# Attention and two expert layers on one core: an earlier column of shares, the first six products on ScalarE, sums of x spread over attention steps

## Chip, core and metric

The kernel runs on one core of one Trainium2 chip. The metric is the device time of one execution in microseconds; the time before is the median of three runs. Engines: TensorE (PE, with its weight loads, PEld), VectorE (DVE), ScalarE (ACT), GpSimd (POOL) and SyncE (SP), which issues most of the transfers.

## What is computed

Causal windowed attention with ALiBi-like distances (2 batches, 8 heads, 768 rows, 64 wide) gives x of 1536 x 512. A first expert layer mixes all 8 experts with shares from 8 Sinkhorn steps; a second gives each token to one expert, by rank and with a capacity of 192. This change is about the end of the attention and the start of the first expert layer:

```python
def _moe_ref(x, w_gate, w1, w2):
    logits = x @ w_gate
    logits = logits - logits.max()
    P = np.exp(logits)
    for _ in range(8):
        P /= P.sum(1, keepdims=True) + 1e-09
        P /= P.sum(0, keepdims=True) + 1e-09
        P *= N / E
    out = np.zeros((N, D), dtype=np.float32)
    for e in range(E):
        h = np.maximum(x @ w1[e], 0.0)
        ye = h @ w2[e]
        out += P[:, e:e + 1] * ye
    return out
```

## The kernel before

There is one program for each engine, written out by hand; an engine runs its instructions in the order in which they are written, and semaphores order them between engines.

**Number format.** Products of the first layer use a high and a low part of each operand (`xhi`, `xlo`, `w1hi`, `w1lo`, `hhi`, `hlo`, `w2hi`, `w2lo`): ScalarE casts the high part, VectorE subtracts it for the low part, and `three` on TensorE issues three matmuls (L1561 to L1563) per product.

**Attention.** `attend_window` on each engine is a loop over 48 steps (`STEPS`; 8 heads, 6 row tiles) and seven more that drain it. In step s TensorE makes the scores of s, transposes the probabilities of s-2 and multiplies those of s-3 by v. VectorE adds the bias and takes the row maximum (L1119, `sc`), ScalarE does exp (L711) and copies the transposed probabilities (`pt`, L718). In every third step VectorE also divides finished rows (`x_rows`, L1049 to L1055), and at fixed steps TensorE transposes x and ScalarE copies it (`x_copy`, L655). In the last steps the three engines already prepare the first expert: `w1_sums`, `x_sums` (L1028 to L1034, four sums of quarters of x, `SUMS`; early ones for half k = 0, the other half after the attention), `x_hi` (L664, ScalarE) and `x_lo` (L1011, VectorE), seven parts (`PARTS`) each. They are the operands of a Strassen-like product: seven products of quarters in place of eight.

**First expert layer.** The 1536 tokens go in two halves (`NS`), each expert's 1024 hidden columns in two units: unit u is one half of one expert. For each unit TensorE computes seven parts of h (`h_part`), then six y blocks of 128 tokens x 512 columns (`y_products`, `TS` = 6), of 12 matmuls each. ScalarE's `period` copies three parts out of PSUM (`part_copy`, L758), casts the seven w1 parts of the next unit (`w1_hi`, L752), takes the relu of h (`h_hi`, L767), and casts w2 (`w2_hi`, L738) once all six y of the unit ahead are in PSUM. TensorE's part 2 waits for the first of these copies (`s_rc`). VectorE's `h_period` and `y_period` do the sums and low parts and multiply each y by its token's share and add it (`y_add`, L1168 for the first unit of a token half, L1170 else).

**The y banks.** The y blocks alternate between two PSUM banks (`Y_BANKS` = 6 and 7). Before y k TensorE waits for `s_acc`, which starts at 2 and is raised by each `y_add`: y 0 and y 1 of the first unit are free to go, y 2 waits for the first `y_add`, y 3 for the second.

**Order of the first units.** TensorE does h of unit 0, h of unit 1, y of unit 0, h of unit 2, y of unit 1, and so on. On VectorE the Sinkhorn chain (L1328 to L1337, with a reduction over partitions on GpSimd, L602, in each of its 8 steps) is interleaved with `first_unit`, a generator of the hi/lo work of units 0 and 1: three pieces (`ASIDE`) per Sinkhorn step, and the rest of it behind the last step. Only then does `layer1(0, 0, True, False)` copy the column of shares (`prob_column`, L1238, `prob_e`) and do the first six `y_adds`. On ScalarE the work of unit 1 and 2 is the first turn of a hardware loop (L819).

Of the kernel before, what the change touches and what calls it, by code (L numbers as in the profile page):

```python
# [31 lines left out]
def build(nc, qT, kT, v, n_global, n_local, gate1, gate2, w1, w2, out):  # L32
# [4 lines left out]
    E = NE // 2  # L37
# [14 lines left out]
    TS = SH // P  # L52
# [11 lines left out]
    with ExitStack() as ctx:  # L64
# [578 lines left out]
        def _(act):  # L643
# [52 lines left out]
            def attend_window():  # L696
                act.wait_ge(s_dd, N_WINDOW)

                def bias_page(h):

                    if h >= 2:
                        act.wait_ge(s_sc, 4 + 2 * QT * (h - 1))
                    act.mul(bias8[:, h % 2, 0:5 * P], dist[:, 0, 0:5 * P], slopes[:, h:h + 1]).then_inc(s_b8, 1)

                bias_page(0)
                for s in range(STEPS + 7):
                    if s < STEPS:
                        n = P if s % QT == 0 else 2 * P
                        for b in range(B):
                            act.wait_ge(s_sc, 4 + 2 * s + b + 1)  # L710
                            act.activation(sc3[:, s % 3, b, 0:n], sc3[:, s % 3, b, 0:n], ACT.Exp,  # L711
                                           bias=negmax[:, 2 * (s % 3) + b:2 * (s % 3) + b + 1], scale=-1.0).then_inc(s_P, 1)
                    if 0 <= s - 2 < STEPS:
                        k = s - 2
                        n = B * (P if k % QT == 0 else 2 * P)
                        act.wait_ge(s_T, 3 + k + 1)
                        act.wait_ge(s_pv, k + 1)
                        act.copy(pt[:, k % 2, 0:n], PS[:, 4 + k % 2, 0:n]).then_inc(s_PT, 1)  # L718
                    if s < STEPS and s % QT == 2 and s // QT + 1 < H:
                        bias_page(s // QT + 1)  # L720
                    if s in XT_STEP:
                        x_copy(*XT_STEP[s])
                    if STEPS - 5 <= s < STEPS - 5 + PARTS:
                        x_hi(0, s - (STEPS - 5), True)
                w2_hi(0, 0)
                x_copy(H // 2 - 1, 0, XBANK_LAST)
                x_copy(H // 2 - 1, 1, XBANK_LAST)
                x_hi(0, 0)
                x_copy(H // 2 - 1, 2, XBANK_LAST)
# [16 lines left out]
            def w1_hi(i, u, n):  # L746

                if n == 0:
                    act.wait_ge(s_raw1[u % 2], i * 16 + 16 * (u // 2 + 1))
                if PART_SUM[n]:  # L750
                    act.wait_ge(s_wsum, of_unit(i, SUMS, u, PART_SUM[n]))
                act.copy(w1hi[:, n], w1_parts(u % 2)[n]).then_inc(s_w1h, 1)  # L752
# [7 lines left out]
            def h_hi(i, u, q):  # L760
# [5 lines left out]
                    act.wait_ge(s_pd, of_unit(i, PARTS, u, PARTS))  # L766
                act.activation(hhi[:, u % 2, fs, ts], h_quarter(u, q), ACT.Relu).then_inc(s_hh, 1)  # L767

            def period(i, u, more, x=None):

                part_copy(i, u, 0, 0)
                part_copy(i, u, 1, 1)
                part_copy(i, u, 2, 2)
                for q in range(4):
                    if more and q < 3:
                        w1_hi(i, u + 1, q)
                    h_hi(i, u, q)
                for n in range(3, PARTS):
                    if more:
                        w1_hi(i, u + 1, n)  # L780
                if x is not None:
                    for n in range(PARTS):
                        x_hi(x, n)
                w2_hi(i, u)

            def layer1(c, i, last):
# [28 lines left out]
                h_hi(0, 0, q)  # L815
            for n in range(3, PARTS):
                w1_hi(0, 1, n)
            for c in range(NS):
                with act.Fori(0, E - 1) as i:  # L819
                    layer1(c, i, False)  # L820
                layer1(c, E - 1, True)

# [90 lines left out]
        def _(dve):  # L913
# [188 lines left out]
            def attend_window():  # L1102
                window_tables()
                qk_lo_first()
                for s in range(STEPS + 7):
                    j, t = s // QT, s % QT
                    if s % HT == 0 and 2 * HT <= s < STEPS + 2 * HT:
                        m = s // HT - 2
                        dve.wait_ge(s_pv, HT * (m + 1) + 2)
                        if m >= 8:  # L1110
                            dve.wait_ge(s_X, (m // 4 - 1) * NC)
                        x_rows(m // 4 % 2, m // 4, m // 2 % 2, m % 2)
                    if s < STEPS:
                        a, n = window(t)[0], window(t)[1] - window(t)[0]
                        for b in range(B):
                            dve.wait_ge(s_S, 2 * s + b + 1)
                            dve.wait_ge(s_b8, j + 1)
                            dve.wait_ge(s_T, s + 1)
                            V.tensor_tensor_reduce(  # L1119
                                out=sc3[:, s % 3, b, 0:n], in0=PS[:, 2 * (s % 2) + b, 0:n],  # L1120
                                in1=bias8[:, j % 2, a:a + n], scale=-0.125, scalar=3.0e38, op0=ALU.add, op1=ALU.min,
                                accum_out=negmax[:, 2 * (s % 3) + b:2 * (s % 3) + b + 1]).then_inc(s_sc, 1)
                        if t == 0 and 0 < j < H - 1:
                            dve.sem_inc(s_qfree, 1)
                    if STEPS - 8 <= s < STEPS - 4:
                        if s == STEPS - 8:
                            dve.wait_ge(s_b8, H)
                            dve.wait_ge(s_ql, 2 * H - 2)
                        w1_sums(0, 0, s - (STEPS - 8))
                    if s == STEPS - 4:  # L1130
                        for n in range(SUMS):
                            x_sums(0, n, True)
                    if STEPS - 3 <= s < STEPS - 3 + PARTS:
                        x_lo(0, s - (STEPS - 3), True)
                    if STEPS <= s < STEPS + 7:
                        w1_lo(0, 0, s - STEPS)

# [103 lines left out]
            def layer1(c, i, first, last):  # L1241

                u = c * UNITS + 1
                end = last and c == NS - 1
                if not (first and c == 0):
                    for _ in h_period(i, u, not end):
                        pass
                    prob_column(c, i)
                    ys = y_adds(c, i, u - 1, first)
                    if end:  # L1250
                        for k in range(FC):
                            next(ys)
                            w2_lo(i, u, k)
                    for _ in y_period(i, u, not end, c + 1 if last and not end else None, ys):
                        pass
                else:
                    prob_column(c, i)
                    for _ in y_adds(c, i, 0, True):
                        pass
                if end:  # L1260
                    for _ in y_adds(c, i, u, False):
                        pass
                else:
                    for _ in h_period(i, u + 1, True):
                        pass
                    if first and c + 1 < NS:
                        for n in range(SUMS):
                            x_sums(c + 1, n)
                    for _ in y_period(i, u + 1, True, None, y_adds(c, i, u, False)):
                        pass  # L1270
# [56 lines left out]
            for it in range(SINK):  # L1327
                ch.step(V.tensor_reduce(red12[:], sink[:, 0:NT, :], AX.X, ALU.add), f"rs{it}", SINK_AT)  # L1328
                ch.step(V.reciprocal(red12b[:], red12[:]), f"rr{it}", SINK_AT)
                ch.step(V.tensor_tensor(shares, shares, red12b[:].unsqueeze(2).to_broadcast([P, NT, E]), ALU.mult),  # L1330
                        f"pm{it}", SINK_AT)
                ch.step(V.tensor_reduce(red8[:], sink[:, :, 0:E].rearrange("p t e -> p e t"), AX.X, ALU.add), f"cs{it}", SINK_AT)
                for _ in range(ASIDE):
                    next(aside, None)
                dve.wait_ge(s_par, 2 + it)
                ch.step(V.reciprocal(red8[:], red8b[:]), f"cr{it}", SINK_AT)
                ch.step(V.scalar_tensor_tensor(shares, shares, float(N // E), red8[:].unsqueeze(1).to_broadcast([P, NT, E]),  # L1337
                                               ALU.mult, ALU.mult), f"cm{it}", SINK_AT)
            for _ in aside:
                pass  # L1340
            for c in range(NS):
# [595 lines left out]
```

## Time and profile before

| | us |
|---|---|
| median of 3 runs | 1413.57 |
| lowest, highest run | 1413.27, 1424.87 |
| profiled execution | 1407.47 |
| its span, first to last instruction | 1405.6 |
| TensorE busy in the span | 1346.3 (96%) |
| VectorE busy | 854.0 (61%) |
| ScalarE busy | 538.8 (38%) |
| mean granted TensorE clock | 0.977 |

All positions below are microseconds from the start of the span of this one profiled execution. Busy times are those of engine instructions; the starts of overlapped instructions stand closer together than their durations. A "granted clock" of 1.00 is 2.4 GHz, 0.50 is 1.2 GHz, and a value between them is a slice in which it changed. "[4.74 <-DVE acc L1168]" behind an instruction says that its engine stood idle for 4.74 us ahead of it, until VectorE's instruction of line 1168 released it.

### The profile page before, as it was taken

To read this page: it belongs to the slowest core of one execution; us is meant where nothing else is said; L and a number is where in the kernel's file an instruction comes from. 1 tells how busy PE (TensorE), PEld (TensorE's weight loads), DVE (VectorE), ACT (ScalarE), POOL (GpSimd) and SP (SyncE) were. 2 spreads that over 40 slices of the span, in tenths; PEclk is the share of its full clock that TensorE was granted. 3 is DMA by queue.
4 is the path that set the end of the run, shared out by engine and by line. 5 is a ranking of instruction groups with operands and counts; after the bars stand their busy time and mean duration, and the time that the engine had idled before them with its cause. 6 is when DMAs were issued, how large, how long until landed. Compare 5 with 4: busy or idle time off the path is not lost.

```text
span 1405.6 us, 21176 instructions
## 1 busy us (share of the span) xinstructions
PE 1346.3 (96%) x7802; PEld 1215.0 (86%) x7802; DVE 854.0 (61%) x1898; ACT 538.8 (38%) x940; POOL 95.4 (7%) x112
## 2 busy tenths in 40 slices
PE   8999799999999999999999999999999965999997
PEld 5887688999998889999888999988899845889997
DVE  5559766656666665686666656666666446886000
ACT  5776233333343333353333333343333112444421
POOL 5651000000000000000000000000000000102101
PEclk9999899999999999999999999999999985999999
DMA  8751011111122111112211111122112014775530
GB/s 187 183 144 62 30 61 60 60 60 60 60 92 87 60 60 60 60 61 75 105 60 60 60 60 60 63 104 71 60 60 75 31 45 138 259 258 167 190 107 23
DMA packets 92569, 125.57 MB, mean 89 GB/s; under 512 B 37216, under 2 KB 43360, under 8 KB 92512
## 3 DMA queue, kind: packets, MB, share of 16 engines
q1 hardware_dynamic: 90464, 118.53, 25.8%
q0 software_dynamic: 2048, 6.29, 1.5%
q8 instruction: 34, 0.56, 0.2%
q14 instruction: 23, 0.19, 0.0%
HBM read 118.52 MB, written 6.29 MB: 89 GB/s over the span
## 4 chain that ended last, share of the span: by engine, by line
PE 88%; DVE 6%; ACT 2%; issue 1%; POOL 1%; DMA 1%; SPq 0%; DVEq 0%; POOLq 0%
PE PS L1561 23%; PE PS L1563 23%; PE PS L1562 23%; PE PS L1860 6%; PE PS L1843 5%; PE PS L1693 2%; DVE G L1467 1%; PE PS L1674 1%; PE PS L1664 1%; PE PS L1890 1%; ACT sc L711 1%; DVE hlo L1160 1%; PE PS L1539 1%; DVE w1lo L1005 0%; PE PS L1818 0%
## 5 line engine op out<-in xcount | busy, mean ns | idle before, releaser
L1561 PE MATMUL PS<-xhi,w1hi 128*128 128x384 f32 x896 | 301.5, 336 | 5.2 <-ACT h_sum L758 4.2
L1563 PE MATMUL PS<-xhi,w1lo 128*128 128x384 f32 x896 | 300.8, 336 | 0.0
L1562 PE MATMUL PS<-xlo,w1hi 128*128 128x384 f32 x896 | 300.7, 336 | 0.0
L1561 PE MATMUL PS<-w2hi,hhi 128*128 128x512 f32 x744 | 291.8, 392 | 7.6 <-DVE acc L1168 4.7
L1562 PE MATMUL PS<-w2lo,hhi 128*128 128x512 f32 x744 | 291.7, 392 | 0.0
L1563 PE MATMUL PS<-w2hi,hlo 128*128 128x512 f32 x744 | 291.6, 392 | 0.0
L1170 DVE SCALAR_TENSOR_TENSOR acc<-PS,prob_e,acc 128x512 f32<-128x512 f32 x180 | 134.9, 750 | 162.6 <-PE PS L1563 162.6
L738 ACT CAST w2hi<-raw 128x2048 fp32r<-128x2048 f32 x31 | 59.3, 1912 | 372.6 <-PE PS L1563 372.6
L1561 PEld LDWEIGHTS PS<-xhi,w1hi 128*128 128x128 f32 x896 | 169.0, 189 | 7.9 <-ACT h_sum L758 4.5
L1561 PEld LDWEIGHTS PS<-w2hi,hhi 128*128 128x128 f32 x744 | 140.8, 189 | 37.0 <-DVE acc L1168 5.2
L1562 PEld LDWEIGHTS PS<-xlo,w1hi 128*128 128x128 f32 x896 | 169.1, 189 | 1.2
L1563 PEld LDWEIGHTS PS<-xhi,w1lo 128*128 128x128 f32 x896 | 168.9, 189 | 0.0
L1563 PEld LDWEIGHTS PS<-w2hi,hlo 128*128 128x128 f32 x744 | 140.6, 189 | 29.5
L1562 PEld LDWEIGHTS PS<-w2lo,hhi 128*128 128x128 f32 x744 | 140.8, 189 | 28.7
L767 ACT ACTIVATE hhi<-h_sum 128x768 fp32r<-128x768 f32 x96 | 81.4, 848 | 136.2 <-DVE h_sum L1154 136.2
L758 ACT COPY h_sum<-PS 128x768 f32<-128x768 f32 x96 | 76.8, 801 | 87.2 <-PE PS L1563 86.9
L1154 DVE TENSOR_TENSOR h_sum<-PS,h_sum 128x768 f32<-128x768 f32 x96 | 91.7, 956 | 26.2 <-PE PS L1563 26.0
L1160 DVE SCALAR_TENSOR_TENSOR hlo<-h_sum,hhi 128x768 fp32r<-128x768 f32 x96 | 91.4, 952 | 1.6
L1005 DVE TENSOR_TENSOR w1lo<-w_sum,w1hi 128x512 fp32r<-128x512 f32 x128 | 85.0, 684 | 0.1
L752 ACT CAST w1hi<-w_sum 128x512 fp32r<-128x512 f32 x124 | 76.0, 613 | 20.9 <-DVE w_sum L996 20.5
L1145 DVE TENSOR_TENSOR w2lo<-raw,w2hi 128x512 fp32r<-128x512 f32 x124 | 82.3, 685 | 1.2 <-ACT w2hi L738 1.2
L988 DVE TENSOR_TENSOR w_sum<-raw 128x512 f32<-128x512 f32 x32 | 22.2, 695 | 97.9 <-PE PS L1563 97.9
(237 smaller groups left out, 1607.9 us busy)
## 6 DMA issues: line engine op xcount, KB each, us to landing
raw<-in_w SPq DMA_DIRECT2D x64, 1024.0 KB, 5.6
expert_weights<-in_w SPq DMA_DIRECT2D x10, 2048.0 KB, 11.6
raw<-in_w SPq DMA_DIRECT2D x3, 2048.0 KB, 8.0
first_expert_w<-in_w SPq DMA_DIRECT2D x3, 2048.0 KB, 14.4
vs<-in_v SPq DMA_DIRECT2D x16, 192.0 KB, 3.1
x_rows<-acc SPq DMA_DIRECT2D x2, 1536.0 KB, 7.9
vw<-in_v SPq DMA_DIRECT2D x16, 120.0 KB, 3.0
qs<-in_qT SPq DMA_DIRECT2D x4, 384.0 KB, 3.8
```

Source lines behind the costliest of these rows:

```text
L752: act.copy(w1hi[:, n], w1_parts(u % 2)[n]).then_inc(s_w1h, 1)
L758: act.copy(h_sum[:, u % 2, fs, ts], part_psum(u, at)).then_inc(s_rc, 1)
L767: act.activation(hhi[:, u % 2, fs, ts], h_quarter(u, q), ACT.Relu).then_inc(s_hh, 1)
L1005: V.tensor_tensor(w1lo[:, W1_SLOT[n]], w1_parts(u % 2)[n], w1hi[:, n].bitcast(F32), ALU.subtract).then_inc(s_w1l, 1)
L1145: ins = V.tensor_tensor(lo[:, k], raw2[:, k], hi[:, k].bitcast(F32), ALU.subtract)
L1154: V.tensor_tensor(h_quarter(u, q), part_psum(u, at), h_quarter(u, q), ALU.add).then_inc(s_c, 1)
L1160: V.scalar_tensor_tensor(hlo[:, u % 2, fs, ts], h_quarter(u, q), 0.0, hhi[:, u % 2, fs, ts].bitcast(F32), ALU.max, ALU.subtract).then_inc( ...
L1170: V.scalar_tensor_tensor(acc[:, t, :], PS[:, Y_BANKS[k % 2], :], prob_e[:, t:t + 1], acc[:, t, :], ALU.mult, ALU.add).then_inc(s_acc, 1)
L1561: T.matmul(o, whi, xh, start=first, stop=False, skip_group_check=shared)
L1562: T.matmul(o, whi, xl, start=False, stop=False, skip_group_check=shared)
L1563: return T.matmul(o, wlo, xh, start=False, stop=last, skip_group_check=shared)
L1860: ins = T.matmul(PS[:, 5 + n % 2, 0:CAP], e_w2[k % 3][:, f, d * P:(d + 1) * P], hT[f], start=f == 0, stop=f == 2 * FC - 1)
```

## The change

Three edits. In the attention, the four early sums of x go from one step (44) to one in each of the steps 44 to 47; the early high parts begin in step 44 instead of 43 and the early low parts in step 46 instead of 45. The column of shares for the first expert is copied directly behind the last Sinkhorn step, ahead of what is left of `first_unit`. The six multiplications of the first unit's y by their shares go from VectorE to ScalarE, behind the casts of w1 for unit 2 and ahead of the cast of w2 (`first_y`); for this ScalarE's first loop turn is written out ahead of the loop.

```diff
@@ ScalarE, attend_window
-                    if STEPS - 5 <= s < STEPS - 5 + PARTS:
-                        x_hi(0, s - (STEPS - 5), True)
+                    if STEPS - 4 <= s < STEPS - 4 + PARTS:
+                        x_hi(0, s - (STEPS - 4), True)
@@ ScalarE, first expert layer
+            def first_y(k):
+
+                if k == 0:
+                    act.wait_ge(s_pe, 1)
+                act.wait_ge(s_y, k + 1)
+                act.mul(acc[:, k, :], PS[:, Y_BANKS[k % 2], :], prob_e[:, k:k + 1]).then_inc(s_acc, 1)
@@ ScalarE, period
+                if isinstance(i, int) and (i, u) == (0, 1):
+                    for k in range(TS):
+                        first_y(k)
                 w2_hi(i, u)
@@ ScalarE, the loop over experts
+            layer1(0, 0, False)
             for c in range(NS):
-                with act.Fori(0, E - 1) as i:
+                with act.Fori(1 - c, E - 1) as i:
                     layer1(c, i, False)
@@ VectorE, attend_window
-                    if s == STEPS - 4:
-                        for n in range(SUMS):
-                            x_sums(0, n, True)
-                    if STEPS - 3 <= s < STEPS - 3 + PARTS:
-                        x_lo(0, s - (STEPS - 3), True)
+                    if STEPS - 4 <= s < STEPS - 4 + SUMS:
+                        x_sums(0, s - (STEPS - 4), True)
+                    if STEPS - 2 <= s < STEPS - 2 + PARTS:
+                        x_lo(0, s - (STEPS - 2), True)
@@ VectorE, layer1
-                else:
-                    prob_column(c, i)
-                    for _ in y_adds(c, i, 0, True):
-                        pass
@@ VectorE, behind the Sinkhorn loop
+            prob_column(0, 0)
             for _ in aside:
                 pass
```

## Rows read from the trace of the kernel before

**Rows 1.** Busy by stage: length, then PE, PEld, DVE, ACT, POOL, clock, DMA, GB/s.

```profile
122.00:163.00 41.00, 35.79 (x188) 33.85 (x183) 38.79 (x89) 19.06 (x30) 6.79 (x9) 0.92 0.20 65
163.00:176.00 13.00, 8.27 (x25) 6.25 (x24) 6.85 (x12) 0.62 (x1) 0.00 (x0) 0.74 0.00 0
176.00:650.00 474.00, 471.18 (x2365) 426.85 (x2364) 310.99 (x451) 174.77 (x239) 0.00 (x0) 1.00 0.19 67
```

**Rows 2.** Waits of PE, 100 to 240 us: us in total, times, longest.

```profile
PE PS L1561 <- DVE acc L1168: 4.7, 1, 4.7
PE PS L1561 <- ACT h_sum L758: 4.2, 1, 4.2
PE PS L1561 <- DVE acc L1170: 2.8, 1, 2.8
PE PS L1693 <- ACT pt L718: 1.8, 2, 1.6
PE PS L1561 <- DVE h_sum L1154: 1.0, 1, 1.0
```

**Rows 3.** VectorE in order of time: start, us, operation; the end of the Sinkhorn chain.

```profile
160.67 0.26 DVE L1337 SCALAR_TENSOR_TENSOR sink<-sink,red 128x96 f32<-128x96 f32 x1
...
162.71 0.68 DVE L996 TENSOR_TENSOR w_sum<-raw,w_sum 128x512 f32<-128x512 f32 x1
...
167.52 0.17 DVE L1238 COPY prob_e<-sink 128x12 f32<-128x12 f32 x1
167.72 1.41 DVE L1168 TENSOR_SCALAR acc<-PS,prob_e 128x512 f32<-128x512 f32 x2
```

**Rows 4.** TensorE in order of time, y of unit 0.

```profile
163.40 0.39 PE L1563 MATMUL PS<-w2hi,hlo 128*128 128x512 f32 x1
168.53 0.80 PE L1561 MATMUL PS<-w2hi,hhi 128*128 128x512 f32 x1 [4.74 <-DVE acc L1168]
...
174.55 0.39 PE L1563 MATMUL PS<-w2hi,hlo 128*128 128x512 f32 x1
...
182.05 0.39 PE L1563 MATMUL PS<-w2hi,hlo 128*128 128x512 f32 x1
```

**Rows 5.** One-microsecond slices, columns as in rows 1; the granted clock is third from the end.

```profile
106.00:107.00 1.00, 0.00 (x0) 0.00 (x0) 1.00 (x6) 1.00 (x3) 0.09 (x1) 1.00 0.00 0
...
167.00:168.00 1.00, 0.00 (x0) 0.00 (x0) 0.96 (x3) 0.00 (x0) 0.00 (x0) 0.79 0.00 0
...
205.00:206.00 1.00, 0.67 (x2) 0.58 (x3) 1.00 (x3) 0.00 (x0) 0.00 (x0) 0.56 0.00 0
```

**Rows 6.** VectorE in order of time, attention steps 44, 45 and 47.

```profile
102.45 0.55 DVE L1028 TENSOR_TENSOR x_sum<-acc 128x384 f32<-128x384 f32 x1
...
105.34 0.41 DVE L1119 CUSTOM_DVE_ANT_0 sc<-PS,bias 128x256 f32<-128x256 f32 x1
...
109.36 0.42 DVE L1119 CUSTOM_DVE_ANT_0 sc<-PS,bias 128x256 f32<-128x256 f32 x1 [1.62 <-PE PS L1664]
```

**Rows 7.** ScalarE in order of time, units 0 to 2.

```profile
143.82 0.62 ACT L752 CAST w1hi<-w_sum 128x512 fp32r<-128x512 f32 x1 [3.82 <-DVE w_sum L996]
144.34 1.49 ACT L758 COPY h_sum<-PS 128x768 f32<-128x768 f32 x2
...
163.42 0.62 ACT L752 CAST w1hi<-w_sum 128x512 fp32r<-128x512 f32 x1 [0.64 <-DVE w_sum L996]
182.47 1.91 ACT L738 CAST w2hi<-raw 128x2048 fp32r<-128x2048 f32 x1 [18.44 <-PE PS L1563]
184.58 0.80 ACT L758 COPY h_sum<-PS 128x768 f32<-128x768 f32 x1 [0.20 <-PE PS L1563]
```

**Rows 8.** Two lines on ScalarE: ns min/median/max, first and last start, form.

```profile
L655 ACT COPY acc<-PS x12: 579/586/592, 46.1 to 118.9; 128x512 f32<-128x512 f32 x12
L703 ACT ACTIVATE bias<-dist,slopes x8: 825/828/831, 12.8 to 90.9; 128x640 f32<-128x640 f32 x8
```

**Rows 9.** Waits of GpSimd, 100 to 115 us, columns as in rows 2.

```profile
POOL red8b L596 <- issue: 5.5, 1, 5.5
```

## The prediction

> **What bounds the kernel now.** I read first the table of busy time by stage [rows 1]. From 176 to 650 us TensorE is busy for 471.18 of 474 us at full clock: there the kernel is bound by TensorE, and what the other engines do costs nothing as long as it comes in time. The two stages ahead are different. From 122 to 163 us TensorE works 35.79 of 41 us while VectorE works 38.79, and from 163 to 176 TensorE works 8.27 of 13 us at a mean granted clock of 0.74. So whatever this change is worth must be found before 176 us, and once TensorE is in its long stage, a shift of it should carry through to the end unchanged.
>
> Next I read who kept TensorE waiting between 100 and 240 us [rows 2]. The longest wait, 4.7 us, is for the first multiplication of a y by its share (`acc` L1168); then 4.2 us for a copied quarter of h (L758), 2.8 us for `acc` L1170, 1.8 us in attention for `pt` (longest single one 1.6), and 1.0 us for a sum of h. The change touches the first and the fourth directly.
>
> The first one, in the order of the work: the last step of the Sinkhorn chain starts at 160.67 us on VectorE, so the shares are final at about 160.9. The column of shares is taken from them only at 167.52, behind 6.9 us of hi/lo work, and the first two multiplications start at 167.72 [rows 3]. TensorE has written y 0 and y 1 into the two y banks; its last matmul of y 1 starts at 163.40, and y 2 must wait until one bank is read: it starts at 168.53 [rows 4].
>
> This wait costs more than itself. The mean granted clock is 0.79 in the slice from 167 us, after more than 3 us of standing still [rows 5], which is the fall from 2.4 to 1.2 GHz. From the matmul at 168.53 to the one at 174.55 are 14 steps in 6.02 us, 0.430 each; from 174.55 to 182.05 are 33 in 7.50 us, 0.227 each [rows 4]. The 14 steps would take 3.18 us at full clock, so the slow stretch costs 2.84 us. Wait and slow stretch together: the pitch at full clock would have put y 2 at 163.63, so 4.90 + 2.84 = 7.74 us stand behind this one late column.
>
> **The change, part by part.**
>
> *Sums of x, one per attention step.* VectorE now does all four back to back, the first at 102.45; one takes 0.55 us, about 0.5 from start to start [rows 6]. Behind them stand the softmax inputs of step 45, which start only at 105.34; from them hang ScalarE's exp, the copy of `pt`, and TensorE's 1.6 us wait [rows 2, 6]. With one sum ahead of it instead of four, that step starts three times 0.5 us earlier (103.8). The wait of TensorE vanishes and TensorE runs about 1.6 us earlier. VectorE does the same amount of work, so it gains only what it idles less. It waits 1.62 us before 109.36 for the scores of step 47 [rows 6]; these come 1.6 us earlier. But the last sum and one part of x now stand behind this point, 2 x 0.5 us, and a later wait of some 0.3 us on TensorE is filled by them: 1.6 - 1.0 + 0.3 = 0.9 us. From there to 163 us VectorE is the engine with no room [rows 1], so 0.9 us is what passes on, not 1.6. The rest comes back as a wait before unit 1's first product, from 1.0 to about 1.7 us; the 4.2 us wait stays as long as it is, since both of its ends hang on VectorE's chain. Bounds: 0 (the steps get in each other's way) and 1.6 (all the idle time goes).
>
> *x parts one step later* (ScalarE's casts and VectorE's lows): same instructions, one step later. The cast of w2 queued behind them has room, since the next copies on ScalarE need TensorE's transposes, which themselves come after the attention. Cost 0; if that room were gone, one step's cast, at most the 0.5 us of a sum of the same shape [rows 6].
>
> *Column of shares ahead of the rest.* The copy moves from 167.52 to about 160.9 - 0.9 = 160.0. With its own wait it takes 0.20 us (167.52 to 167.72) [rows 3], and all that is queued behind it on VectorE slides by 0.20, among it the last sum of w1 at 162.71, for which ScalarE's last cast before the multiplications waits.
>
> *Multiplications on ScalarE.* Six instructions leave VectorE (750 ns each) [rows 3], which saves nothing there, because VectorE is idle between them. On ScalarE they stand behind the cast that starts at 163.42 and takes 0.62 [rows 7]. New start: 163.42 + 0.62 - 0.9 + 0.2 = 163.34. The trace shows no multiplication of this shape on ScalarE. Nearest rows: a copy of 128x512 from PSUM into the same tensor, 586 ns, and a multiplication by a column, 128x640, 828 ns [rows 8]. These are the bounds; between them I take 0.68, the copy plus a tenth of a microsecond for reading the scale, since shape and source are the copy's. So y 0 is out at 164.02, and with the 0.06 us that the hand-over takes now (167.72 + 0.75 to 168.53 [rows 3, 4]) TensorE starts y 2 at 164.08 instead of 168.53: 4.45 us earlier (the 0.9 from above is in it). Its own wait is then 164.08 - (163.63 - 0.9) = 1.35 us. y 3 needs y 1's multiplication, which follows at once, 2 us ahead of need.
>
> The Trainium skill (ScalarE: Activation LUTs, "Rules for kernel authors") says a multiplication belongs on VectorE, not ScalarE, which speaks against this part; the comparison it gives is for bf16. The rows here (586 ns for the copy on ScalarE against 750 for the product on VectorE) do not bear it out for this shape. By its figure for an activation with one pointer operand ("What ACT_TABLE_LOAD costs") my estimate from the page is 0.19 + 0.09 + 512 x 0.00083 = 0.71 us, and the sum would change by 0.03.
>
> *Clock.* Does it still fall? It stayed at 1.00 through the 1.6 us wait (slice 106 to 107), and had fallen by the end of the 2.8 us wait (0.56 in the slice from 205) [rows 5, 2]. 1.35 us is nearer to the first. I take: no fall, 2.84 us saved.
>
> *What is late next.* The cast of w2 (182.47) and the first copy of the next unit (184.58) now stand behind the sixth multiplication on ScalarE [rows 7]. They come 0.68 us later relative to TensorE. TensorE needs that copy only when it begins its third part, 4.2 us after the last y; the copy is ready 2.1 + 0.8 = 2.9 us after it, now 3.6. Cost 0, 0.6 us to spare. The unrolled first turn of ScalarE's loop adds instructions to its code, none to its work: 0. The 2.8 us wait for `acc` L1170 near 205 us has a different cause (eight sums of the next x on VectorE) and stays.
>
> **Sum.** 4.45 + 2.84 = 7.3 us. The profiled execution takes 1407.47 us (span 1405.6) and should become 1400.2. The median of the three runs is 1413.57, 6.1 above the profiled one; the same difference gives 1406.3. That is 0.5%, less than the 1% that a measurement of this kernel can tell from no change.
>
> **The rivals.**
>
> A: *the clock falls at y 2 all the same.* The wait is only shortened, and a wait of 2.8 us did bring a fall [rows 5]. Against it: 1.6 us did not. Then the 2.84 us stay: 1409.2. The Trainium skill (TensorE: Matmul & The Clock Gate, "What's actually happening") adds that the moment of a change varies with the phase of a counter that runs on by itself; by that rule the falls behind the 2.8 and 4.2 us waits may also move by one or two microseconds either way.
>
> B: *more than forecast.* All of the 1.6 us passes on and the slow stretch behind the 2.8 us wait is not entered (about 7 steps x 0.2 = 1.4 us): 1413.57 - 7.3 - 0.7 - 1.4 = 1404.2.
>
> C: *the change does not do what it says:* y 2 is held by something else that was hidden behind the column, say ScalarE still casting w1 until 167. Its casts end at 164.04 [rows 7], which speaks against it. Then only 0 to 0.9 us are won: about 1413.
>
> D: *slower.* ScalarE's unrolled turn is new straight code, with a loop behind it. If entering new code halts the engine, the one long wait for nothing visible in this stretch is the measure, 5.5 us on GpSimd [rows 9]. It would fall once ahead of unit 1's first copy, straight into TensorE's path, and once at the loop, less the 1.2 us that copy has to spare: 5.5 + 4.3 - 7.3 = +2.5, 1416.1. It decides from about 4.3 us per entry. Against it: ScalarE enters its loop today between the cast at 143.82 and the copy at 144.34, and nothing is lost between them [rows 7].
>
> **How the numbers follow.** Forecast 0.66, A 0.14, B 0.09, C 0.07, D 0.04. The bounds of the unknown costs give 1406.3 - 0.7 - 0.1 to 1406.3 + 0.9 + 0.15, thus 1405.5 to 1407.4. To take in A and B with their uncertainty by 1 us, I give 1403.6 to 1410.4; left out are C and D, about 1 in 10, and some scatter between runs. Faster by over 1% would need 14 us, that is all the waits of [rows 2] at once: 0.03. Slower by over 1%: 0.02. Within 1%: 0.95.
>
> **What would show it.** `prob_e` at about 160 us; six `acc` rows on ScalarE, 0.6 to 0.8 us each, the first near 163.3; TensorE's wait for y 2 at 1 to 1.6 us with a clock of 1.00 around it; no 1.6 us wait at 105 us; the wait before unit 1's first product longer than 1.0 us; the wait for `acc` L1170 still near 2.8 us. The forecast is wrong if the long stage of TensorE starts less than 6 or more than 9 us earlier, or if new waits appear in it.

## The result and the profile after

| | before, us | changed, us |
|---|---|---|
| median of 20 runs | 1413.55 | 1405.31 |
| lowest, highest | 1410.08, 1428.78 | 1403.99, 1424.68 |
| profiled execution (span) | 1407.47 (1405.6) | 1403.99 (1402.1) |

The ratio is 0.9921 with a 95% interval of 0.9896 to 0.9946. The forecast time, 1406.3, is within 1 us of the median. But I had called 0.5% less than a measurement can tell from no change, and this one, good to 0.25% either way, tells it: the gain is 0.54% to 1.04%, or 7.6 to 14.7 us. The 7.3 us of my sum lie just below that, and the middle of the interval, 11.2 us, is half as much again.

The table of busy time by stage, changed kernel (length, then PE, PEld, DVE, ACT, POOL, clock, DMA, GB/s), answers to [rows 1]:

```profile
122.00:163.00 41.00, 35.48 (x181) 33.59 (x179) 38.86 (x89) 18.58 (x29) 6.79 (x9) 0.92 0.17 56
163.00:169.00 6.00, 5.29 (x24) 4.29 (x24) 3.73 (x7) 2.03 (x4) 0.00 (x0) 1.00 0.00 0
169.00:640.00 471.00, 468.17 (x2351) 424.23 (x2350) 307.38 (x446) 176.54 (x242) 0.00 (x0) 1.00 0.20 67
```

The stage of 13 us at a clock of 0.74 is gone; in its place TensorE is busy for 5.29 of 6 us at 1.00. Ahead of it nothing has changed much: VectorE is still without room. The waits of TensorE from 100 to 240 us, changed kernel, answer to [rows 2]:

```profile
PE PS L1568 <- ACT h_sum L758: 4.2, 1, 4.2
PE PS L1568 <- DVE acc L1180: 2.8, 1, 2.8
PE PS L1568 <- DVE h_sum L1164: 1.3, 1, 1.3
...
PE PS L1568 <- ACT acc L774: 0.7, 1, 0.7
PE PS L1700 <- ACT pt L718: 0.3, 2, 0.2
```

The wait of 4.7 us for y 2 is one of 0.7 us for ScalarE's product, that of 1.6 us in attention is gone, and the one ahead of unit 1's first product has grown from 1.0 to 1.3. The other two are as they were.

Where it happens, on VectorE, ScalarE and TensorE in order of time (answer to [rows 3, 7, 4]):

```profile
159.59 0.26 DVE L1343 SCALAR_TENSOR_TENSOR sink<-sink,red 128x96 f32<-128x96 f32 x1
159.89 0.17 DVE L1248 COPY prob_e<-sink 128x12 f32<-128x12 f32 x1
...
161.84 0.69 DVE L1007 TENSOR_TENSOR w_sum<-raw,w_sum 128x512 f32<-128x512 f32 x1
```

```profile
162.56 0.62 ACT L752 CAST w1hi<-w_sum 128x512 fp32r<-128x512 f32 x1 [0.85 <-DVE w_sum L1007]
163.08 1.26 ACT L774 ACTIVATE acc<-PS,prob_e 128x512 f32<-128x512 f32 x2
166.88 0.69 ACT L774 ACTIVATE acc<-PS,prob_e 128x512 f32<-128x512 f32 x1 [2.54 <-PE PS L1570]
...
175.62 1.90 ACT L738 CAST w2hi<-raw 128x2048 fp32r<-128x2048 f32 x1
177.42 0.80 ACT L758 COPY h_sum<-PS 128x768 f32<-128x768 f32 x1
```

```profile
162.72 0.39 PE L1570 MATMUL PS<-w2hi,hlo 128*128 128x512 f32 x1
163.82 0.50 PE L1568 MATMUL PS<-w2hi,hhi 128*128 128x512 f32 x1 [0.71 <-ACT acc L774]
...
174.61 0.39 PE L1570 MATMUL PS<-w2hi,hlo 128*128 128x512 f32 x1
```

y 2 starts at 163.82 instead of 168.53, and the 47 steps from there to the last matmul of y 5 at 174.61 take 10.79 us, 0.230 each: full speed throughout. The column moved 7.6 us, from 167.52 to 159.89.

In some executions (the profiles of e1, e2, e4 and e5) TensorE works without a pause from 18 to 62 us and the granted clock is still 0.50, which puts everything behind that some 18 us later; so positions in other runs are given from a mark, the first early sum of w1 on VectorE (93.31 in the kernel before, 93.22 in the changed one).

### The profile page after: what moved, and what is told of

It reads as the page before. It is cut to its first block, busy times and chain, and to the rows that moved or that the text cites. A ratio compares the mean times of both kernels' runs of the same rounds, so it can differ in the third digit from the quotient of the medians.

```text
span 1402.1 us, 21150 instructions
## 1 busy us (share of the span) xinstructions
PE 1344.4 (96%) x7802; PEld 1213.3 (87%) x7802; DVE 849.5 (61%) x1892; ACT 542.4 (39%) x946; POOL 95.3 (7%) x112
## 4 chain that ended last, share of the span: by engine, by line
PE 88%; DVE 6%; ACT 2%; issue 2%; POOL 1%; DMA 1%; SPq 0%; DVEq 0%; POOLq 0%
PE PS L1568 23%; PE PS L1570 23%; PE PS L1569 23%; PE PS L1867 6%; PE PS L1850 5%; PE PS L1700 2%; DVE G L1474 1%; PE PS L1671 1%; PE PS L1681 1%; PE PS L1897 1%; DVE hlo L1170 0%; DVE xlo L1022 0%; PE PS L1825 0%; ACT sc L711 0%; PE PS L1833 0%
```

## The experiments

For each run I read the same things from its trace, all in us. A slow stretch is one with a granted clock of 0.50. "y 2" is the start of the third y of unit 0, counted from the mark. "Wait" is TensorE's wait there, and "wait, unit 1" its wait for the third y of unit 1. "Slow" is what the slow stretch behind such a wait costs: from the first matmul of that y to the last of the unit's sixth, less 47 steps of 0.227 us. D is the distance from the mark to the second store of x (SyncE, line 487 before, at 1132.60), and the tail is the rest of the span.

| run | y 2 | wait | slow | wait, unit 1 | slow, unit 1 | D | tail |
|---|---|---|---|---|---|---|---|
| before | 75.2 | 4.7 | 2.9 | 2.8 | 1.6 | 1039.3 | 273.0 |
| before again (e9) | 78.3 | 5.1 | 2.0 | 2.8 | 0.1 | 1040.1 | 278.4 |
| changed | 70.6 | 0.7 | 0.1 | 2.8 | 1.8 | 1032.1 | 276.8 |
| changed again (e5) | 70.6 | 1.5 | 0.1 | 2.8 | 1.7 | 1032.1 | 281.4 |
| changed, third (e10) | 70.7 | 1.5 | 0.1 | 2.8 | 1.8 | 1032.2 | 277.1 |
| sums only (e1) | 74.2 | 5.1 | 1.7 | 2.8 | 0.2 | 1035.7 | 273.3 |
| column and products only (e2) | 72.9 | 1.5 | 0.1 | 2.8 | 1.8 | 1034.4 | 272.2 |
| column only (e3) | 75.2 | 4.4 | 1.6 | 2.8 | 0.1 | 1036.5 | 273.0 |
| two products on VectorE (e4) | 70.0 | 0.3 | 0.3 | 2.8 | 1.7 | 1031.6 | 273.3 |
| next x later (e6) | 70.6 | 1.5 | 0.1 | none | 0 | 1027.4 | 277.4 |
| y 2 later by four products (e7) | 73.5 | 3.7 | 1.7 | 2.8 | 0.1 | 1034.9 | 277.0 |
| y 2 later by two products (e11) | 72.0 | 3.0 | 1.7 | 2.8 | 0.1 | 1033.5 | 280.1 |
| all three (e8) | 70.0 | 0.6 | 0.2 | none | 0 | 1026.8 | 277.9 |

e1 to e4 ran in one session on one chip, e5 to e8 in a second session on another, e9 to e11 in a third on yet another. (The wait of e4 is the distance between two matmuls less their usual pitch.)

The wait at y 2 differs between executions of the changed kernel (0.7, 1.5 and 1.5) while y 2 itself stays at 70.6 or 70.7. The slow stretch behind the 4.2 us wait makes the difference. All 13 profiles have one there (behind 3.8 us in e8), for 6.8 us in six and for 3.4 us in seven. The same 8 us in the changed kernel and in e10 (granted clock third from the end):

```profile
143.00:151.00 8.00, 6.88 (x23) 6.88 (x24) 7.45 (x21) 3.08 (x5) 1.78 (x2) 0.57 0.04 4
```

```profile
143.00:151.00 8.00, 6.76 (x31) 6.76 (x32) 7.48 (x20) 3.21 (x5) 1.78 (x2) 0.79 0.05 8
```

Behind the long one TensorE comes to y 2 some 0.8 us later and waits 0.8 us less, since y 2 is set by VectorE's and ScalarE's work: there the length of the stretch costs nothing.

**Sums only.** Of the diff, the two hunks in `attend_window` alone.

> Only the sums of x are spread over the attention steps; column and products of y stay on VectorE as before. My theory (0.9 us passes on, since VectorE has no room from 110 to 167 us): first product of unit 1 about 0.9 us earlier than before, y 2 of unit 0 at 167.6 instead of 168.53 with the clock still falling, second store of x (line 487, at 1132.60 before) at about 1131.7; time 0.9 us below before, not measurable in the total. Rival (all of TensorE's 1.6 us passes on): 1131.0. Rival (the order of the sums is worth nothing at all): 1132.6.

Ratio 0.995 (0.9917 to 0.9983): 2 to 12 us, where I had expected 0.9 and nothing measurable. y 2 starts 1.0 us earlier than before, as my theory said (0.9), not 1.6. D is 3.6 us shorter, not 0.9: the other 2.6 us are slow stretches, 2.9 to 1.7 behind y 2 and 1.6 to 0.2 in unit 1. The edit does not touch the instructions there, and the same kernel gives other lengths too (before and e9), so the length of a slow stretch is not a property of the kernel alone. That was the first sign that my 2.84 us was one draw of several.

**Column and products only.** The diff without its hunks in `attend_window` (the column early, the six products on ScalarE).

> The column is early and the six products are on ScalarE, but the sums of x stay in one attention step. My theory (the two edits are independent and add up, 7.3 = 0.9 + 6.4): y 2 starts at about 164.7, clock 1.00 around it, second store of x at 1126.2, time about 6.4 us below before. Rival (the two parts need each other, because a longer wait at y 2 brings the fall of the clock back): y 2 at 164.7 but slow matmuls behind it, store at 1129.

Ratio 0.9968 (0.9934 to 1.0001). No fall of the clock at y 2, behind a wait of 1.5 us. But y 2 comes only 2.3 us earlier than before, not 3.8: this execution had a slow stretch in attention, behind the wait of 1.6 us that the sums make. I come back to it under e9. D is 4.9 us shorter, not 6.4: 2.3 at y 2, 2.7 for the slow stretch behind it, and 0.1 lost in unit 1. The ratio's interval just reaches 1.

**Column only.**

```diff
@@ before, VectorE
                 else:
-                    prob_column(c, i)
                     for _ in y_adds(c, i, 0, True):
                         pass
...
+            prob_column(0, 0)
             for _ in aside:
                 pass
```

> Only the column of shares is early; the six products stay on VectorE behind the rest of the hi/lo work of units 0 to 2, sums in one step. My theory (the column was not the last thing in the way, the order on VectorE was): the first product stays at 167.72, y 2 at 168.53, store of x at 1132.6, time as before. Rival (the late column alone costs the 7.7 us): y 2 at about 163.7 and the store at 1125.

Ratio 1.0012 (0.9979 to 1.0044): no change that the runs can tell, and y 2 where it was, as my theory said. VectorE in order of time, column only:

```profile
160.88 0.17 DVE L1238 COPY prob_e<-sink 128x12 f32<-128x12 f32 x1
...
167.65 1.40 DVE L1168 TENSOR_SCALAR acc<-PS,prob_e 128x512 f32<-128x512 f32 x2
```

The column is ready at 161 and the products still wait until 167.65. A late column was the outward sign; the seven low parts of w1 ahead of the products were the thing in the way. Its D, 2.8 us shorter than before with y 2 at the same place, is again slow stretches alone (1.6 for 2.9, and 0.1 for 1.6).

**Two products on VectorE.** Sums spread and column early as in the changed kernel; no ScalarE product. The rest of the edit, against the kernel before:

```diff
@@ VectorE, first_unit
                 w1_sums(0, 2, 3)
                 yield
+                for k in range(2):
+                    y_add(0, 0, 0, k, True)
+                    yield
                 for n in range(PARTS):
                     w1_lo(0, 2, n)
                     yield
@@ VectorE, layer1
-                    for _ in y_adds(c, i, 0, True):
-                        pass
+                    for k in range(2, TS):
+                        y_add(c, i, 0, k, True)
```

> Sums spread and column early as in the changed kernel, but all products stay on VectorE: the first two are put directly behind the last sum of w1 and ahead of the seven low parts of w1 for unit 2, the other four behind them. If ScalarE was only a means to come ahead of that work (my theory): first product at about 162.4 to 162.5, y 2 at 163.2 to 163.3, some 0.5 us earlier than in the changed kernel (163.82), store of x at 1124.8, time equal to or half a microsecond below the changed kernel, some 8 us below before. Rival (VectorE has no room, and its seven low parts 1.4 us later hold up the next unit): store at 1126 or later.

Ratio 0.9919 (0.9886 to 0.9952), y 2 at 70.0 against 70.6, D 0.5 us below the changed kernel. So ScalarE was a means, not the cause: what counts is that two products come ahead of the low parts. VectorE can give them without harm to the next unit.

**All runs of the first session.** One profile of a kernel says little about how its executions scatter, so here are all their times, in us:

| kernel | 1.6 us wait in attention | lowest group | middle group | above |
|---|---|---|---|---|
| before | yes | 16, 1404.8 to 1410.1 | 12, 1415.8 to 1417.4 | 2 |
| column only (e3) | yes | 8, 1404.5 to 1410.2 | 3, 1416.5 to 1417.3 | 1 |
| column and products only (e2) | yes | 6, 1401.0 to 1404.6 | 5, 1410.6 to 1412.8 | 1 |
| sums only (e1) | no | 10, 1403.5 to 1406.6 | none | 2 |
| two products on VectorE (e4) | no | 7, 1398.2 to 1400.3 | none | 1 |

The few above are the late starts of the result section. The middle group, 9 to 10 us above the lowest, has 20 of 54 executions of the kernels with the wait and none of 20 of those without it. Its mean granted clock is 0.971 to 0.974, against 0.975 to 0.980 in the lowest group of the same kernels, so most of the time is lost to a lower clock. In the other two sessions the kernel before scatters over more than 13 us without such clear groups, and the changed kernel, its late starts aside, stays within 5 us but for one execution in each (1410.8 and 1412.2). Without the late starts, the mean of the kernel before is 1411.1 and that of sums only 1405.1. The sums are worth 6.0 us here, 1.8 of them in the lowest group and the rest because there is no middle one. Where the slow stretches of a middle execution lie isn't known: no profile is of one.

**The changed kernel again, and the tail.**

> The changed kernel as it is, a second time, beside the others. D stands for the distance from the first early sum of w1 on VectorE to the second store of x, 1039.3 us before and 1032.1 in the changed kernel; the tail from that store to the end was 273.0 and 276.8. Profiles of four variants showed that a wait of 2.8 us is followed by slow matmuls in some executions and not in others. Theory (gain = 4.6 us of waits that is there in every execution + a slow stretch of 1.4 to 2.8 us that depends on when the clock falls and returns): D between 1030.6 and 1033.5, the wait at y 2 again 0.7 with a clock of 1.00; tail 272 to 277. Rival (the 3.8 us longer tail belongs to the change): tail again above 276.

D 1032.05 against 1032.06: the changed kernel's stage up to the store is the same to a hundredth. The wait at y 2 was 1.5 us, though, and not 0.7 again. Ratio 0.9942 (0.9904 to 0.998). The rival, a longer tail, was still alive here, since the tail was even longer (281.4). Up to 3.4 us of that are a slow stretch of 6.8 us from 1284 us on (e11 has one of 3.4 us, from 1227), which the other profiles lack. The run of the kernel before in the third session speaks to the rival.

> The kernel before, a second time, with its profile, beside the changed kernel. D is the distance from the first early sum of w1 to the second store of x, the tail the rest of the span behind that store. All five profiles of variants that ran in one session had a tail of 272.2 to 273.3, all of another 276.8 to 281.3, with 3.6 and 5.0 us to the landing of a gathered block of x rows. Theory (the tail goes with the chip and session, not with the change; its wait for y 2 is always there, its slow stretches are 3.4 or 7 us long): wait at y 2 of 4.7 to 5.2 us, D between 1036 and 1039.3, tail the same within 1.5 us as that of the changed kernel of this call. Rival (the change makes the tail longer): tail of this run about 4 us shorter than that of the changed kernel.

> The changed kernel, a third time, in the same call as the kernel before. Theory: D 1032 within 1, no fall of the clock at y 2 whether its wait is 0.7 or 1.5 us, tail as in the run beside it within 1.5 us; D of the two kernels differs by 4.6 to 7.3 us and the times by the same. Rival: tail 4 us longer than that of the kernel before, and the times differ by less than D does.

On one chip, in one session: tail 278.4 for the kernel before and 277.1 for the changed one. In the first session all of e1 to e4 have 272.2 to 273.3, those with the parts of the change too. So the longer tail does not belong to the change. In the issues of transfers of the two first profiles, before and then changed (x count, median us from issue to landing), the gathers of rows of x are the likely difference. The other profiles that have this figure go the same way (3.3 to 3.5 in e1 to e4, 5.1 and 5.2 in e5, e6 and e11). That the gathers make the tail longer is argued, not shown:

```profile
acc<-x_rows,tid POOLq DMA_INDIRECT x16, 3.6
```

```profile
acc<-x_rows,tid POOLq DMA_INDIRECT x16, 5.0
```

This also explains why the first two profiles differ by only 3.5 us: SyncE's second store of x is 7.32 us earlier, and 3.8 us go in a tail that depends on the chip and session. SyncE in order of time, before and changed:

```profile
1132.60 0.37 SPq L487 DMA_DIRECT2D x_rows<-acc  x1
```

```profile
1125.28 0.37 SPq L487 DMA_DIRECT2D x_rows<-acc  x1
```

The ratio of the third session is 0.992 (0.9883 to 0.9957) for the changed kernel and 0.9996 (0.995 to 1.0041) for the kernel before against itself. D of the kernel before, 1040.1, lies above the 1036 to 1039.3 that I expected, and the difference of the two, 7.9, above the 4.6 to 7.3.

e9 shows one more thing. One-microsecond slices of the kernel before, second profile, and TensorE's row at the end of the attention wait:

```profile
106.00:107.00 1.00, 0.00 (x0) 0.00 (x0) 1.00 (x6) 1.00 (x3) 0.01 (x1) 1.00 0.00 0
107.00:108.00 1.00, 0.72 (x4) 0.72 (x5) 0.79 (x3) 1.00 (x4) 0.41 (x1) 0.74 0.00 0
108.00:109.00 1.00, 1.00 (x7) 1.00 (x7) 0.00 (x0) 0.92 (x3) 0.00 (x0) 0.50 0.00 0
...
107.28 0.54 PE L1693 MATMUL PS<-vw,pt 128*128 128x65 f32 x2 [1.63 <-ACT pt L718]
```

The same wait of 1.63 us as in [rows 2], and here the clock falls behind it and stays at 0.50 for about 7 us. The first h part after attention comes 2.8 us later from the mark than in the first profile, and y 2 3.1 us later. Of the four profiles with this wait (before, e2, e3, e9) two had a fall: e9 at once, and e2 2.2 us behind the end of the wait, for 3.4 us. The nine without the wait had none there.

**How long a wait brings a fall at y 2.** In `first_y`, ahead of the first product (`range(2)` in e11):

```diff
+                if k == 0:
+                    for m in range(4):
+                        act.mul(acc[:, k, :], PS[:, Y_BANKS[k % 2], :], prob_e[:, k:k + 1]).then_inc(s_rep, 1)
+                        act.wait_ge(s_rep, m + 1)
```

> Changed kernel, but ScalarE does the first product four times more, each waited for, so y 2 is released about 4 x 0.7 = 2.8 us later: TensorE's wait there goes from 0.7 to 3.5 us. It measures rival A's condition, whether and for how long the clock falls behind such a wait. If a wait of this length brings a fall whenever it comes (by the rows of before: 4.7 us did), slow matmuls stand behind it for 3 to 7 us and D is 2.8 + 1.4 to 2.8 above the changed kernel, about 1036.3 to 1037.7. If the clock stays, D is 1034.9. The repeats change nothing in the result.

> Changed kernel with the first product done twice more on ScalarE, each waited for: y 2 comes 1.4 us later, TensorE's wait there is 2.1 to 2.9 us. With the wait of 3.7 us (four repeats) the clock fell for about 3.4 us. Theory (a fall needs the standing still to be long, and 2 us is not; the waits of 2.8 us seen so far had a fall in six of nine profiles): no fall if the wait is 2.1, either if it is 2.9. D about 1033.5 without a fall, 1034.9 with one. Rival (any standing still above 1.6 us brings it): fall.

TensorE's row and the slices around y 2, four repeats:

```profile
166.79 0.50 PE L1573 MATMUL PS<-w2hi,hhi 128*128 128x512 f32 x1 [3.74 <-ACT acc L779]
...
166.00:167.00 1.00, 0.21 (x1) 0.21 (x2) 0.83 (x2) 0.97 (x3) 0.00 (x0) 1.00 0.00 0
167.00:168.00 1.00, 1.00 (x4) 0.77 (x4) 0.00 (x0) 0.32 (x1) 0.00 (x0) 0.59 0.00 0
168.00:169.00 1.00, 1.00 (x4) 0.81 (x3) 0.00 (x0) 0.00 (x0) 0.00 (x0) 0.50 0.00 0
```

The clock fell in both, for about 3.4 us (1.7 us lost), not 7. D is 1034.9 and 1033.5, though: 2.9 and 1.4 us above the changed kernel, which is the delay alone, because the slow stretch of unit 1 was missing in both. I had expected D from 1036.3 with a fall at four repeats, and 1034.9 with one at two; both missed. At y 2, all seven profiles with a wait of 0.3 to 1.5 us kept the clock, and all six with 3.0 to 5.1 lost it. The 2.8 us wait of unit 1 had a slow stretch in six profiles and none in five, and it was missing wherever there had been one of 3.4 us behind y 2. In all five profiles with this wait and a clock kept at y 2 it was there. So the two places have to be added up: 4.5 us in the first profile of the kernel before, but 1.7 to 2.1 in the other five with a fall at y 2, and 1.8 to 2.0 in the five without one.

**The next wait removed.** The eight sums of the next half of x (`x_sums(c + 1, n)`) go behind `y_period` of unit 1.

```diff
                     for _ in h_period(i, u + 1, True):
                         pass
-                    if first and c + 1 < NS:
-                        for n in range(SUMS):
-                            x_sums(c + 1, n)
                     for _ in y_period(i, u + 1, True, None, y_adds(c, i, u, False)):
                         pass
+                    if first and c + 1 < NS:
+                        for n in range(SUMS):
+                            x_sums(c + 1, n)
```

> Changed kernel, and the eight sums of the second half of x go from ahead of y 0 of unit 1 to behind its last low parts on VectorE, where it is idle. Theory: the wait of 2.8 us for acc near 198 us goes, with the slow stretch of 1.4 us where it is there: D 2.8 to 4.2 us below the changed kernel, about 1028 to 1029; time 3 to 4 us below the changed kernel of this call. Rival (the sums now hold up w1 of the next unit): D falls by less than 2 us and a new wait of about 1 us stands near 220 us.

Ratio 0.9886 (0.9852 to 0.992), median 1399.98 against 1407.21 for the changed kernel in the same session; D 4.7 us shorter, 0.5 more than the most I had expected (3.0 of wait and 1.7 of slow stretch). The lowest times, 1399.58 and 1404.32, differ by 4.7 too; the medians, of six and eight runs, differ by more. VectorE in order of time, next x later:

```profile
206.76 1.02 DVE L1039 TENSOR_TENSOR x_sum<-acc 128x384 f32<-128x384 f32 x2
...
210.63 0.68 DVE L999 TENSOR_TENSOR w_sum<-raw 128x512 f32<-128x512 f32 x1
212.45 0.69 DVE L1002 TENSOR_TENSOR w_sum<-raw,w_sum 128x512 f32<-128x512 f32 x1 [1.14 <-PE PS L1570]
```

The sums now take 3.9 us behind the last low part, and the idle 1.14 us behind them show that VectorE is not late there; no new wait of TensorE appears.

**All three.** e6, with the two products of e4 in place of ScalarE's, and on ScalarE `part_copy(0, 1, 0, 0)` and `part_copy(0, 1, 1, 1)` ahead of the last `w1_hi(0, 1, n)`.

> The changed kernel with three more moves: first two products back on VectorE directly behind the last sum of w1 (as in the earlier run), the other four behind the low parts; sums of the next x later; on ScalarE the first two copied quarters of h of unit 1 ahead of the last cast of w1 of unit 1, for which it waits 3.8 us. Theory: -0.5 (products) -2.8 to -4.2 (sums) -0.7 (part 2 of unit 1 then waits for its low part of w1, ready 0.7 us before the copy) -> D about 1026.5 to 1028, time 4 to 5.5 us below the changed kernel. Rival (VectorE's chain sets everything before 163 us, so the copies gain nothing): D 0.7 higher.

Ratio 0.988 (0.9847 to 0.9914), median 1399.67: with e6 the best of the second session; the two can't be told apart. D is inside what I had expected, but not for the reason given. It is 0.54 us shorter than in e6; y 2 is 0.62 earlier, so all of it is the products and the copies gave nothing. TensorE's waits, all three:

```profile
PE PS L1575 <- DVE w1lo L1017: 3.8, 1, 3.8
PE PS L1575 <- DVE h_sum L1165: 1.2, 1, 1.2
```

The 4.2 us wait for a copy, as in the changed kernel, has become one of 3.8 us for a low part of w1 on VectorE, and what TensorE wins there it loses again at y 2, which hangs on VectorE. The rival was right.

## Why the prediction was right or wrong

*Sums, 0.9 us passed on.* This is the term that failed. What it says of y 2 is right, which moved 1.0 us in e1; the wait ahead of unit 1's first product grew to 1.0 to 1.4 us and not to 1.7. VectorE in order of time, changed kernel, answer to [rows 6]:

```profile
102.38 0.56 DVE L1039 TENSOR_TENSOR x_sum<-acc 128x384 f32<-128x384 f32 x1
...
103.80 0.41 DVE L1130 CUSTOM_DVE_ANT_0 sc<-PS,bias 128x256 f32<-128x256 f32 x1
...
107.82 0.42 DVE L1130 CUSTOM_DVE_ANT_0 sc<-PS,bias 128x256 f32<-128x256 f32 x1 [1.13 <-PE PS L1671]
```

Step 45 starts at 103.80, as computed, and step 47 at 107.82 instead of 109.36. The step that failed is that I priced the 1.6 us wait as idle time alone (bounds 0 to 1.6), since the clock stayed at 1.00 through it. It did in the profile I had; in two of four it does not, and y 2 then comes 3.1 us later (e9). And the edit takes away the middle group of executions: the runs of the first session put it at 6.0 us, and e1's interval at 2 to 12. The runs show how much; which slow stretches make up the middle group stays open.

*Column on VectorE, 0.20 us.* Right: 159.89 to 160.09, and the last sum of w1 came 0.87 us earlier than before (0.7 forecast).

*Products on ScalarE.* 0.68 us was forecast; the six of them, by line (ns min/median/max):

```profile
L774 ACT ACTIVATE acc<-PS,prob_e x6: 679/690/691, 163.1 to 175.0; 128x512 f32<-128x512 f32 x6
```

The estimate from the Trainium skill (ScalarE: Activation LUTs, "What ACT_TABLE_LOAD costs") was 0.71, nearly as close. The comparison that speaks for VectorE in the Trainium skill (the same page, "Rules for kernel authors") is for bf16, and these fp32 rows don't bear it out: 690 ns on ScalarE against 750 [rows 3]. But e4 agrees with the advice to use VectorE for another reason, the order of work there. y 2 started at 163.82 where I had 164.08, since the first product overlapped the cast ahead of it (163.08, not 163.34).

*No fall of the clock at y 2.* Right in seven of seven profiles with 0.3 to 1.5 us. Its worth, 2.84 us, was mis-sized too, the other way: over the six profiles that have such a stretch the loss was 2.9, 2.0, 1.7, 1.7, 1.7 and 1.6. And the slow stretch of unit 1, which I held constant, is 1.6 to 1.8 or nothing: it was missing in five of those six and there in all five with a clock kept at y 2. In e9 against e10 the clock at these two places together is worth 0.3 us, not 2.84. The Trainium skill (TensorE: Matmul & The Clock Gate, "What's actually happening") has the moment of the change run-dependent. These profiles agree: the clock fell 1.0 us ahead of y 2 in one profile of the kernel before and 2.8 us ahead in the other. In the prediction I used it for a rival and not for the terms of the sum.

*Nothing late behind it, loop entry free.* Right. The cast of w2 at 175.62 starts behind the sixth product, and no wait appears in the long stage. Of rivals A to D none came as described, though the median, 1405.3, lies between the forecast's 1406.3 and B's 1404.2.

*What can be told from no change.* I took 1% for it and gave no working. With 20 runs of each kernel the interval is 0.25% to either side, so even the 7.3 us of my sum (0.52%) could be told.

*The sum.* (Rival A's time is 1409.1 by its own terms, not 1409.2.) 7.3 us by my sum, 7.2 by D in the first pair of profiles, 7.9 in e9 against e10. That the first agrees so well is partly chance: 4.62 at y 2 (4.7 from the start of the span, 4.45 forecast), 2.73 behind it, -0.12 in unit 1. In e9 against e10 it is 7.6 at y 2, of which 3.1 come from the fall in attention, and 0.3 behind it. The medians differ by 8.2 us and the ratio says 7.6 to 14.7. The rest is in executions that neither profile shows: 6 of the 20 of the kernel before lie at 1421 us and above, and 2 of the 20 of the changed one. The middle group of the first session, found with the wait in attention alone, is the likely reason; for these 20 it is argued, since the clock of the kernel before is not on record for them.

*Measured against profiled.* I carried the 6.1 us between profiled execution and median over unchanged. It became 1.3 us. The profiled execution came out 3.8 us above the 1400.2 that I gave for it, as much as the tail was longer, and the median 1.0 us below its forecast. That the median is so close is therefore luck: two errors, of 3.8 and 4.8 us, cancel.

## What to carry to other kernels

When an engine waits for a value, look at what stands in the queue between the value and its first use: moving the column alone gave nothing, and the products ahead of seven other instructions gave 3.6 us at y 2 on ScalarE and 4.2 us on VectorE, both against sums only. A wait on TensorE has two prices, the wait and the clock behind it; the second is a draw, so bound it by several stretches of several profiles and not by the one at hand, and ask whether a fall taken away here lets the next wait have one. Look at the times of all executions before trusting one profile: a second group of times is a cost that it may not show. Compare stages by marks near their ends: here three profiles of the changed kernel agreed within 0.2 us from mark to mark, while their spans differed by 22.

## What was not expected of the hardware

A wait of only 1.63 us, in attention, was followed by a fall of the granted clock from 1.00 to 0.50 in two of four profiles, once for 3.4 and once for 6.8 us. At y 2 waits up to 1.5 us never were, in seven profiles, and waits of 3.0 us and more always, in six. The slow stretches behind the waits of this stage come in these two lengths, and the same instructions in the same kernel got either.
